# A fused retention, mixture-of-experts and rational feed-forward kernel: routing tables and flag loads moved into the expert loop, the last tokens' tail reordered

## The reference

```python
logits = x @ w_gate                      # x: 1536 x 512, w_gate: 512 x 8
expert_idx = np.argmax(logits, axis=1)
probs = np.exp(logits - logits.max(-1, keepdims=True)); probs /= probs.sum(-1, keepdims=True) + 1e-09
gate_w = probs[np.arange(N), expert_idx]
...
h = np.maximum(np.einsum('ecd,edf->ecf', disp, w1), 0.0)
y = np.einsum('ecf,efd->ecd', h, w2)
...
out[i] = gate_w[i] * y[expert_idx[i], pos[i]]
...
out = (P(x @ w_in) / Q(x @ w_in)) @ w_out   # P, Q: polynomials of each element; x is now the mixture's result
```

## Time and profile before

| | |
|---|---|
| median of 3 runs | 542.57 us |
| the profiled execution | 542.48 us |
| its span, first to last instruction | 540.7 us |
| PE busy | 530.9 us (98%) |
| DVE, ACT, POOL busy | 424.1, 335.1, 78.3 us |
| granted TensorE clock | 1.000 |

### The profile page before, as it was taken

How to read it: one execution, slowest core, us unless ns; L and a number is a source line. 1 busy time by engine, 2 the same in 40 slices (tenths; PEclk the granted TensorE clock), 3 DMA queues, 4 the chain that set the end, 5 groups by cost and what they waited for, 6 DMA issues and landing times.

```text
span 540.7 us, 8567 instructions
## 1 busy us (share of the span) xinstructions
PE 530.9 (98%) x3127; PEld 443.9 (82%) x3127; DVE 424.1 (78%) x760; ACT 335.1 (62%) x518; POOL 78.3 (14%) x74
## 2 busy tenths in 40 slices
PE   7999998999999999999999999999999999999997
PEld 5888887888888888888788888888888888888885
DVE  4567778765858568595989999998888888888885
ACT  3556545565846557475968876657667566655552
POOL 3333345600101011003010000004000000200000
PEclk9999999999999999999999999999999999999999
DMA  9999739959986483922160000002000000200002
GB/s 193 226 271 260 234 132 365 357 197 360 384 325 217 173 323 141 375 101 71 41 236 1 1 21 19 1 1 96 22 21 19 1 0 1 79 0 1 0 1 78
DMA packets 65039, 72.26 MB, mean 134 GB/s; under 512 B 41186, under 2 KB 41698, under 8 KB 64996
## 3 DMA queue, kind: packets, MB, share of 16 engines
q1 hardware_dynamic: 59268, 58.08, 34.3%
q0 software_dynamic: 3136, 9.46, 5.4%
q10 hardware_dynamic: 2592, 4.16, 2.1%
HBM read 59.09 MB, written 12.60 MB: 133 GB/s over the span
## 4 chain that ended last, share of the span: by engine, by line
PE 94%; DVE 2%; SPq 1%; DMA 1%; issue 1%; ACT 0%; DVEq 0%; ACTq 0%
PE bank L900 10%; PE bank L902 10%; PE bank L901 10%; PE up_low L901 7%; PE up_low L900 7%; PE up_low L902 7%; PE up_low L906 5%; PE up_high L906 5%; PE up_high L902 4%; PE up_high L901 4%; PE up_high L900 4%; PE up_low L907 3%; PE up_high L907 3%; PE bank L279 2%; PE bank L324 2%; PE bank L313 1%
## 5 line engine op out<-in xcount | busy, mean ns | idle before, releaser
L827 DVE TENSOR_TENSOR T<-raw,T 128x1024 fp32r<-128x1024 f32 x60 | 71.5, 1220 | 36.1 <-ACT T L821 36.1
L821 ACT ACTIVATE T<-raw 128x1024 fp32r<-128x1024 f32 x60 | 60.5, 1070 | 34.9 <-PE bank L902 33.9
L900 PE MATMUL up_low<-x2H,T 128*128 128x512 f32 x176 | 69.3, 394 | 0.0
L902 PE MATMUL up_low<-x2H,T 128*128 128x512 f32 x176 | 68.5, 389 | 0.0
L901 PE MATMUL up_low<-x2L,T 128*128 128x512 f32 x176 | 68.5, 389 | 0.0
L1460 ACT ACTIVATE sq<-up_low 128x512 f32<-128x512 f32 x44 | 26.2, 596 | 64.4 <-PE up_low L902 64.2
L1481 DVE SCALAR_TENSOR_TENSOR wa<-sq,coef,wa 128x512 f32<-128x512 f32 x48 | 35.9, 748 | 28.7 <-ACT wa L1462 28.7
L900 PE MATMUL bank<-T,hL 128*128 128x512 f32 x128 | 50.6, 395 | 0.0
L902 PE MATMUL bank<-T,hH 128*128 128x512 f32 x128 | 49.9, 390 | 0.0
L901 PE MATMUL bank<-T,hH 128*128 128x512 f32 x128 | 49.9, 389 | 0.0
L1474 ACT ACTIVATE rc<-wa,cst 128x512 f32<-128x512 f32 x48 | 34.8, 725 | 20.5 <-DVE wa L1481 15.8
(11 more groups left out here) (199 smaller groups left out, 1247.7 us busy)
## 6 DMA issues: line engine op xcount, KB each, us to landing
raw<-in_moe_w_dram SPq DMA_DIRECT2D x14, 2048.0 KB, 11.0
raw<-in_moe_w_dram SPq DMA_DIRECT2D x8, 512.0 KB, 4.8
w_out_raw<-in_moe_w_out_dram SPq DMA_DIRECT2D x4, 1024.0 KB, 16.6
ybuf<-ysb ACTq DMA_DIRECT2D x15, 256.0 KB, 4.4
qin<-in_q_dram SPq DMA_DIRECT2D x12, 256.0 KB, 5.0
kin<-in_k_dram SPq DMA_DIRECT2D x12, 256.0 KB, 5.3
vin<-in_v_dram SPq DMA_DIRECT2D x12, 256.0 KB, 5.3
xbuf<-xt SPq DMA_DIRECT2D x12, 256.0 KB, 4.2
```

The costliest lines, as they stand in the source:

```text
L821: e.activation(W[w][:, 0, cols], raws[par][:, w, cols], ACT.Copy).then_inc(r.wH[w], 1)
L827: e.tensor_tensor(W[w][:, 1, cols], raws[par][:, w, cols], W[w][:, 0, cols].bitcast(F32), ALU.subtract).then_inc(r.wL[w], 1)
L900: nc.tensor.matmul(out_, aL, bH, start=start, stop=False)
L902: return nc.tensor.matmul(out_, aH, bH, start=False, stop=stop)
```

## The change

The calls of `dve_gates`, `dve_coef`, `dve_gate_sum` and `dve_order` leave the place between tail and experts and are made once, as the last thing of the first expert's step on DVE (`behind_first`). `act_gates` goes to the same step on ACT, ahead of the last output copy. The flag loads of DVE and ACT go into the last expert's step. The wait of the first activation copy for `s_ex` and `s_gate` becomes one for the low parts and the stores of `xbuf`, since `hs` now shares room with `xt`, and the small routing tiles have their own.

In the tail, tile 11's logits are taken in column groups too, in bank 0. PE's order there is new. DVE takes `xL` ahead of the full index and leaves the last half of the first weight split for behind the counts, so the first up-projection waits for the other seven (`s_w0L`), and its third group for all.

```diff
@@ -139,3 +139,6 @@
         w_out_raw = sb(early, "w_out_raw", [P, FT * DM])
-        xt = [sb(early, f"xt{i}", [P, DM]) for i in range(2)]
+        rows = ExitStack()
+        xt = [sb(rows, f"xt{i}", [P, DM]) for i in range(2)]
+        rows.close()
+        hs = [sb(early, f"hs{i}", [P, 2, NMAIN * P]) for i in range(2)]
         small = ExitStack()
@@ -147,3 +150,3 @@
         small.close()
-        hs = [sb(early, f"hs{i}", [P, 2, NMAIN * P]) for i in range(2)]
+        small_room = sb(early, "small_room", [P, TB * P * 2])
         xd = sb(early, "xd", [P, NMAIN, DM])
@@ -328,2 +331,6 @@
 
+        def gate_bank(t):
+
+            return bank[7] if t + 1 < NT else bank[0]
+
         def pe_logits_apart(t):
@@ -332,5 +339,8 @@
             e.wait_ge(s_xT, t + 1)
-            wait(e, s_pc, t)
+            if t + 1 < NT:
+                wait(e, s_pc, t)
+            else:
+                e.wait_ge(s_eq, NT)
             for kk in range(KD):
-                last = e.matmul(bank[7][kk * QG:(kk + 1) * QG, P:2 * P], wg[:, kk, :], xT[t % 2][:, kk, :], start=True,
+                last = e.matmul(gate_bank(t)[kk * QG:(kk + 1) * QG, P:2 * P], wg[:, kk, :], xT[t % 2][:, kk, :], start=True,
                                 stop=True)
@@ -341,11 +351,3 @@
             e.wait_ge(s_lt, t + 1)
-            e.matmul(bank[7][:, 0:E], lgT[:, :], pick[:, :], start=True, stop=True).then_inc(s_lg, 1)
-
-        def pe_logits(t):
-            e = nc.tensor
-            e.wait_ge(s_xT, t + 1)
-            e.wait_ge(s_eq, NT)
-            for kk in range(KD):
-                last = e.matmul(bank[0][:, 0:E], xT[t % 2][:, kk, :], wg[:, kk, 0:E], start=kk == 0, stop=kk == KD - 1)
-            last.then_inc(s_lg, 1)
+            e.matmul(gate_bank(t)[:, 0:E], lgT[:, :], pick[:, :], start=True, stop=True).then_inc(s_lg, 1)
 
@@ -386,3 +388,3 @@
 
-        def pe_x_stored():
+        def pe_x_stored(parts):
 
...
@@ -394,3 +396,3 @@
                                     start=False, stop=False, skip_group_check=True)
-            last.then_inc(main.xt, NMAIN)
+            last.then_inc(main.xt, 1)
 
@@ -469,3 +471,3 @@
             wait(e, s_lg, t)
-            e.tensor_copy(lgT[:, :], bank[7][:, P:2 * P]).then_inc(s_lt, 1)
+            e.tensor_copy(lgT[:, :], gate_bank(t)[:, P:2 * P]).then_inc(s_lt, 1)
 
@@ -475,3 +477,3 @@
             e.wait_ge(s_lg, t + 1)
-            logits = bank[7 if t + 1 < NT else 0][:, 0:E]
+            logits = gate_bank(t)[:, 0:E]
             e.tensor_copy(lg_all[:, t, :], logits).then_inc(s_lc, 1)
@@ -667,11 +669,14 @@
             pe_values(t)
-            pe_x_late(0, range(KD))
+            pe_x_late(0, range(2))
             pe_positions(t - 1)
-            pe_logits(t)
+            pe_x_late(0, range(2, 3))
+            pe_logits_apart(t)
+            pe_x_late(0, range(3, KD))
             pe_rows(t)
-            pe_x_late(1, range(KD // 2))
+            pe_logits_sum(t)
+            pe_x_late(1, range(KD))
             pe_index(t - 2)
-            pe_x_late(1, range(KD // 2, KD))
+            pe_x_stored(range(2))
             pe_positions(t)
-            pe_x_stored()
+            pe_x_stored(range(2, KD))
             pe_x_late(2, range(KD))
@@ -744,3 +749,3 @@
             dve_choose(late)
-            for c in range(late - SPLIT_FROM, 2 * WC):
+            for c in range(late - SPLIT_FROM, 2 * WC - 1):
                 dve_first_half(c)
@@ -757,13 +762,22 @@
             dve_count(late + 1)
+            dve_logits_apart(late + 2)
             dve_put(late)
             dve_choose(late + 2)
+            dve_lane(late + 1)
             dve_place(late + 2)
             dve_fit(2)
-            dve_lane(late + 1)
-            dve_put(late + 1)
             dve_count(late + 2)
+            dve_put(late + 1)
             dve_lane(late + 2)
             dve_put(late + 2)
-            dve_index()
             dve_xL_first()
+            dve_index()
+            dve_crowd()
+            dve_first_half(2 * WC - 1)
+
+        def dve_crowd():
+            e = nc.vector
+            e.wait_ge(s_cnt, 1)
+            e.tensor_reduce(crowd[:, :], bank[7][:, 2 * E:3 * E], AX.X, ALU.max).then_inc(s_flag, 1)
+
 
@@ -920,6 +934,7 @@
             n = r.nt * P
-            e.wait_ge(r.wL[0], (i * 2 + (par + 1)) * WC)
             if first:
+                e.wait_ge(s_w0L, 2 * WC - 1)
                 pe_up_first(r)
             else:
+                e.wait_ge(r.wL[0], (i * 2 + (par + 1)) * WC)
                 e.wait_ge(r.xL, (i * 2 + (par + 1)) * r.nt)
@@ -930,2 +945,4 @@
                     e.wait_ge(s_flag, 1)
+                if first and g == 2:
+                    e.wait_ge(r.wL[0], WC)
                 for f in (2 * g, 2 * g + 1):
@@ -966,4 +983,5 @@
             if isinstance(i, int) and i + par + g == 0:
-                e.wait_ge(s_ex, 1)
-                e.wait_ge(s_gate, 8)
+                e.wait_ge(s_xl, LAST)
+                for t in range(2):
+                    e.wait_ge(s_xst[t], NT // 2 * 16)
             e.activation(hs[g % 2][:, :, 0:n], up_pair[g % 2][:, :, n:2 * n], ACT.Copy).then_inc(r.hH, 1)
@@ -1046,3 +1064,3 @@
 
-        def act_experts(r, split=False, last=None):
+        def act_experts(r, split=False, last=None, behind_first=lambda: None):
             def step(i, par, more):
@@ -1067,2 +1085,4 @@
                     act_y(r, i, par, s)
+                if isinstance(i, int) and i + par == 0:
+                    behind_first()
                 if not more:
...
@@ -1295,2 +1317,13 @@
 
+        def dve_x2L_again(s):
...
@@ -1357,2 +1390,3 @@
             act_split(r, i, par, 1, 1)
+            load_flag()
             act_hH(r, i, par, 0)
@@ -1791,6 +1825,7 @@
             act_xH_first()
-            act_gates()
+            flag = []
 
-            n = crowded(e)
-            act_experts(main, True, act_last_expert)
+            def act_last_step(r, i, par):
+                act_last_expert(r, i, par, lambda: flag.append(crowded(e)))
+            act_experts(main, True, act_last_step, act_gates)
 
...
@@ -1823,10 +1858,14 @@
             dve_last_tiles()
-            e.wait_ge(s_cnt, 1)
-            e.tensor_reduce(crowd[:, :], bank[7][:, 2 * E:3 * E], AX.X, ALU.max).then_inc(s_flag, 1)
-            dve_gates()
-            dve_coef(e)
-            dve_gate_sum()
-            dve_order()
-            n = crowded(e)
-            dve_experts(main, True, dve_last_expert)
+            flag = []
+
+            def dve_weights():
+                dve_gates()
+                dve_coef(e)
+                dve_gate_sum()
+                dve_order()
+
+            def dve_last_step(r, i, par):
+                flag.append(crowded(e))
+                dve_last_expert(r, i, par)
+            dve_experts(main, True, dve_last_step, dve_weights)
 
@@ -1836,6 +1875,6 @@
                 for s in range(TB):
-                    dve_x2L_ready(again, s)
+                    dve_x2L_again(s)
                 for c in range(OREADY):
                     dve_wout_ready(again, c)
-            spilled(e, n, lambda: dve_experts(spill), redo)
+            spilled(e, flag[0], lambda: dve_experts(spill), redo)
             blocks(dve_block)
```

More of the change, by code:

```diff
@@ L385, in pe_index @@
                      start=False, stop=True, skip_group_check=True).then_inc(s_im, 1)
-        def pe_x_stored():
+        def pe_x_stored(parts):
             e = nc.tensor
             e.wait_ge(main.xd, NMAIN * 16)
-            for kk in range(KD):
+            for kk in parts:
                 for s in range(NMAIN):
@@ L757, in dve_last_tiles @@
             dve_count(late + 1)
+            dve_logits_apart(late + 2)
             dve_put(late)
             dve_choose(late + 2)
+            dve_lane(late + 1)
             dve_place(late + 2)
             dve_fit(2)
-            dve_lane(late + 1)
+            dve_count(late + 2)
             dve_put(late + 1)
-            dve_count(late + 2)
             dve_lane(late + 2)
             dve_put(late + 2)
+            dve_xL_first()
             dve_index()
-            dve_xL_first()
+            dve_crowd()
[4 more added lines that the diff above has]
+            e.tensor_reduce(crowd[:, :], bank[7][:, 2 * E:3 * E], AX.X, ALU.max).then_inc(s_flag, 1)
         class Run:
@@ L1073, in act_experts, with dve_experts @@
             experts(nc.scalar, step)
-        def dve_experts(r, split=False, last=None):
+        def dve_experts(r, split=False, last=None, behind_first=lambda: None):
             def step(i, par, more):
@@ L1293, in dve_x2L_ready @@
                             x2s[0][0][:, :, toks].bitcast(F32), ALU.subtract).then_inc(r.x2L, 1)
+        def dve_x2L_again(s):
+            e = nc.vector
+            e.wait_ge(again.x2H, s + 1)
+            toks = slice(s * P, (s + 1) * P)
+            for kk in range(KD):
+                last = e.tensor_tensor(x2s[0][1][:, kk, toks], bank[4 + s][:, kk * P:(kk + 1) * P],
```

(6 more changed lines are left out.)

## The result

The changed kernel takes 550.90 us, the median of 4 runs (550.39 to 551.75). The kernel before took 542.54 us in 4 runs (542.51 to 542.59). The ratio is 1.0156, with a 95% interval of 1.0138 to 1.0173. The profiled execution of the changed kernel took 550.93 us, its span is 549.1 us, and its mean granted clock is 0.991.

A forecast was written before the change was run, and what follows sets the result against it. PE was taken as the bound, with time to gain only ahead of 91 us. Sum: 542.48 - 2.1 (gain) + 10.2 (wait) + 1.9 (slow restart) = 552.5 us; range 547.5 to 554.5, own case 551 to 554.5 at 53%.

The forecast's parts named there:

- the wait: Ahead of the third expert's transposes, PE waits 10.2 us for gathered tokens queued behind POOL's scatters; bounds 6.7 and 11.3.
- the slow restart: After the wait for the third expert's tokens, PE's matmuls run slowly at first, costing 1.9 us; bounds 0 and 3.
- The gain: In the tail and between tail and experts, PE saves 2.1 us in all; bounds 1.2 and 2.6.
- The start of the tail: Ahead of tile 10's logits, moving DVE's last half split away removes PE's 0.26 us wait; bounds 0 and 0.26.
- the logits and the reordering: In the tail, tile 11's logits in column groups save 0.35 us; reordering gives nothing, up to 0.5 either way.
- the failed cover: If PE's work meanwhile does not hide DVE's `lgT` copy, the logits' sum waits and nothing of 0.35 us is left.
- The low parts: Ahead of the products with the low parts, making `xL` before the index removes 0.85 us; bounds 0.5 and 0.85.
- The stretch from their products to the transposes: Between tail and experts, moving gates and flag loads removes PE's 0.66 us wait ahead of the first expert's third group.
- PE at full pace: Rival: the wait for the third expert's tokens comes, but PE resumes without slowdown, 550.6 us; chance 27%.
- The fast scatters: Rival: POOL's scatters issue near their lower bound, wait 6.7 us, total 547.1, or 549.0 with slow start; chance 12%.
- The gather in time: Rival: the third expert's tokens land by 117.5, the moved work is hidden, 540.4 us; chance 5%.
- a tail without its gain: Rival: in the tail PE waits for a fit or low part instead, 553.4 us; chance within the forecast's 53%.

The follow-up runs named there:

- experiment 1: Changed kernel with the third expert's gather moved ahead of the eight scatters in POOL's queue: 539.91 us, ratio 0.9951.
- experiment 9: Kernel of experiment 1 with DVE's last half split of the first weights back ahead of index and counts: 540.16 us, ratio 0.9952.
- experiment 10: Kernel of experiment 1 with tile 11's logits as four matmuls in sequence, without DVE's copy and the sum: 539.89 us, ratio 0.9943.
- experiment 8: Kernel of experiment 1 with the full index again ahead of the low parts on DVE: 540.84 us, ratio 0.9961.
- experiment 3: Changed kernel with SP's four w_out loads held until the third expert's gather has landed: 550.88 us, ratio 1.0151.
- experiment 4: Changed kernel with the fourth expert's last 2 MB weight load and the w_out loads held until the third expert's gather has landed: 548.14 us, ratio 1.0097.
- experiment 5: Changed kernel with ten matmuls of zeros on PE during the wait ahead of the third expert's transposes: 549.03 us, ratio 1.0117.
- experiment 7: Changed kernel with the old tail and logits in sequence, gates and flag loads still behind the first expert: 552.38 us, ratio 1.0172.
- experiment 2: Changed kernel with four scatters ahead of the third expert's gather and four behind it: 539.83 us, ratio 0.9946.

## Why the prediction was right

The forecast was 552.5 us and the measured time is 550.9, within the range of 547.5 to 554.5, but just under the 551 to 554.5 that the forecast's own case was given. The mechanism is the one forecast, at its place, and experiment 1 shows that it is the whole loss. Of the 1.6 us between the two numbers the wait accounts for 1.2, and the last stores, for which the sum has no term, for 0.7; the slow restart pulls the other way by 0.2. The terms, one by one:

**The gain** was put at 2.1 us and is 2.32 at the second expert's transposes. But it comes from other terms than I had. The start of the tail gave 0.37 (0.26 is the wait, experiment 9; 0.11 lies before the tail and is no part of it). From there to the low parts' products PE needed 85.21 - 0.85 - 74.06 = 10.30 us before and 83.95 - 73.69 = 10.26 after, so the logits and the reordering gave 0.04, not 0.35. I had noted the failed cover as a bound. The sum takes no wait here, and experiment 10 shows that the column groups alone gave nothing. Part of the price is the reordering, which I had given nothing: the 16 transposes of stored rows took 81.63 - 79.85 = 1.78 us before, and in two halves take 80.27 - 79.30 = 0.97 and 81.36 - 80.33 = 1.03. The low parts gave the 0.85 in full (experiment 8).

The stretch from their products to the transposes went from 96.54 - 85.21 = 11.33 to 94.22 - 83.95 = 10.27, so 1.06, where I had 0.66. The other 0.40 is in three places. The wait itself cost more than its 0.66, since that idle time counts only from the end of the last matmul, while matmuls under way overlap. The eight pairs ahead of it and the wait took 90.78 - 87.19 = 3.59 us, and the same pairs take 88.66 - 85.89 = 2.77 now, a difference of 0.82. The third group's eight pairs took 93.70 - 90.78 = 2.92 us before, and take 91.43 - 88.66 = 2.77 now, 0.15 less, 0.11 of it at the first matmul behind the wait. The last 0.09 lie in the low parts' products (0.04) and the fourth group (0.05). A missed term of 0.4 made up for one of 0.35 that wasn't there: that the gain came out at 2.3 is luck.

**The wait** was put at 10.2 and is 9.03. Its pieces: `place_all` ends at 105.08, not 105.7, because the four splits start at 98.14, 2.7 us earlier than before and not 2.1. To the first scatter it is 0.79 as forecast. From there to the first gather it is 116.30 - 105.87 = 10.43 us, not 12.15. The gathers are 1.76 apart, not 1.26, and the second lands in 8.40, not 7.9. PE wanted it at 117.47 (117.5). The largest error is that of the scatters, -1.7 us, and the gathers' +0.5 and +0.5 made up for part of it. I had laid the 7.9 us of landing to w_out's loads. Experiments 3 and 4 show that it is the weight load ahead of them, which the kernel before issues at 119.24, just ahead of that gather.

I took the long issues of the earlier trace rows as the price of scatters beside splits. The rows after say when it is paid. The split of 107.38 to 108.61 starts 0.2 us behind the scatter of 107.17, which keeps its 0.98. The gather of 116.30 starts while the split of 115.67 to 116.89 runs, and takes 1.45, until 0.86 behind that split's end. Before it was so too: 93.01 + 2.03 = 95.04 is 0.84 behind a split that ended at 94.20. In both traces an issue that begins inside a split ends 0.81 to 0.94 us after it, and one that begins first is not touched. (One exception at the edge: the scatter of 88.87 begins 0.03 us into a split and takes 1.00.) So what a split costs an issue hangs on how much of the split is left: the scatter of 108.45 begins 0.16 us ahead of its split's end and takes 0.99. It is luck of the phase, and the scatters met the splits late in their run:

```profile
107.38 1.23 DVE L841 TENSOR_TENSOR T<-raw,T 128x1024 fp32r<-128x1024 f32 x1 [2.29 <-ACT T L835]
...
115.67 1.22 DVE L841 TENSOR_TENSOR T<-raw,T 128x1024 fp32r<-128x1024 f32 x1
```

The Trainium skill ("SBUF — State Buffer", Who interferes with whom) has it that a DVE instruction with two inputs in SBUF contends with a GpSimd instruction that reads SBUF, and that the order of issue decides who is held up. These rows agree, as far as an indirect DMA's issue reads its offsets (`place_all`, `index`) from SBUF. The same section's remark that tensor_tensor leaves descriptor writing alone gave 10.0 us for the scatters, near the 10.43, but not for the reason that it names: issues are held up by splits, in both traces, only seldom in this stretch. In the first experiment the scatter of 107.74 begins 0.16 us into the split of 107.58, and takes 1.92.

**The slow restart** was put at 1.9 and is 2.12 (1.9 by experiment 5). I had argued from the pace of the first matmuls, where the clock's column reads 1.00, and not from the clock. The column does show it here, 0.50 from 122. That the number came out near is luck: the comparison was looser than I thought, and behind the same wait of 9.0 us the restart cost 1.74 us in experiment 3 and 2.71 in experiment 7, and behind 4.7 us it cost 2.69 in experiment 4.

**The rivals.** PE at full pace would have been 550.6, and by its time alone it would fit better than the forecast. Rows and experiment 5 refute it: the restart is there, and the time is lower because the wait is shorter and the last stores end sooner. The fast scatters (549.0 with the slow start) were nearer to the truth for the scatters, 10.43 against its 10.0, but took 6.5 us for a landing that was 8.4. The gather in time needed what experiments 1 and 2 make: a gather with no scatters, or only four, ahead of it. The last rival, a tail without its gain, is refuted by the 2.3 us.

**What stays open:** why two groups of transposes take the 0.2 us that tile 11's logits save, why DVE was later in experiment 4's tail, why the restart's cost varies from 1.7 to 2.7 us, and why the last stores end 0.7 us sooner in every changed kernel.

## What to carry to other kernels

When a piece of work moves behind other work, follow who is released by its last instruction and what stands behind that one in the same queue: 2.3 us of DVE instructions moved into a real gap cost 11 us, because two gathers stood behind eight scatters that waited for them. Changing places in POOL's queue gave all of it back, and left the kernel 2.8 us under the one before. Price a transfer by the traffic that will lie beside it, not by the median of its kind. A long wait of PE costs more than its length, here 1.7 to 2.7 us on 9.0, so taking it away pays twice.

## What the runs showed of the hardware

- The time to land of one and the same gather (128 rows by its index) was 3.9 to 4.5 us with the queues nearly empty (experiments 2 and 4) and 8.3 to 9.1 beside a 2 MB load, and there four more loads of 1 MB each behind it made no difference (experiment 3).
- The granted clock fell while PE was idle, from 1.00 to 0.50 (2.4 to 1.2 GHz), and PE came back to its full pace 4.3 us after it had begun to work again (126.50 to 130.82). Behind waits of the same 9.0 us that was 3.7 us in experiment 3 (126.42 to 130.16) and 5.6 in experiment 7 (127.88 to 133.49), and behind 4.7 us of waiting 5.6 in experiment 4. So the length of the wait did not set the length of the slow stretch. Matmuls of zeros in the wait kept the clock at 1.00 (experiment 5).
- A POOL issue of an indirect DMA that begins inside a DVE instruction with both inputs in SBUF ends 0.81 to 0.94 us after that instruction. It takes 0.94 to 0.99 us where little of the instruction is left, and up to 2.03 where it has just begun (within the first 0.03 us some were held up and some not). This holds for the splits (128x1024) and for the low parts of the activations (128x512; 97.08 + 1.09 before, 0.84 behind its end). Issues that begin early in an instruction with one input in PSUM are not held up: 90.17 before begins 0.12 us into the sum of line 977 and takes 0.98.
